# One step per slot: both products of the same 256 rows, with the table look-ups in front of the first

## The reference

```python
for e in range(E):                       # first mixture, E = 8
    mask = e_idx == e
    h = np.maximum(x[mask] @ w1[e], 0.0)         # [rows, 384] @ [384, 1024]
    out[mask] = gate_w[mask, None] * (h @ w2[e]) # [rows, 1024] @ [1024, 384]
...
for e in range(E):                       # second mixture
    for k in range(2):
        mask = top2[:, k] == e
        h = np.maximum(x[mask] @ w1[e], 0.0)
        out[mask] += top2_w[mask, k, None] * (h @ w2[e])
```

## Time and profile before

| | |
|---|---|
| median of 3 runs | 1062.32 us (1060.22 to 1062.54) |
| profiled execution, its own time | 1059.91 us |
| its span, first to last instruction | 1058.2 us |
| PE busy | 922.0 us (87%) |
| DVE, ACT, POOL busy | 529.5 us (50%), 226.3 us (21%), 355.8 us (34%) |
| mean granted TensorE clock | 0.955 of full speed |
| chain that ended last | PE 80%, DVE 10%, issue 6% |

### The profile page before, as it was taken

One profiled execution on the slowest core, in us unless ns is written; L12 is line 12 of the kernel. 1 busy time (PEld: TensorE's weight loads), 2 busy tenths in 40 slices (PEclk: granted clock), 3 DMA queues, 4 the chain that ended last, 5 costly groups with the idle time before them and its releaser, 6 DMA issues.

```text
span 1058.2 us, 22450 instructions
## 1 busy us (share of the span) xinstructions
PE 922.0 (87%) x7279; PEld 885.6 (84%) x7280; DVE 529.5 (50%) x946; ACT 226.3 (21%) x393; POOL 355.8 (34%) x358
## 2 busy tenths in 40 slices
PE   5999998999999987571699899998999999998893
PEld 5888887999999977561599899998989999998893
DVE  8889997863233342248543534335344353433431
ACT  2232251111011121143111313113122221311110
POOL 7333335043221321004443252433424334252321
PEclk9999998999999998875699999999999999999997
DMA  6666872083110111440343343423423434322221
GB/s 235 219 219 221 279 249 68 1 306 121 39 53 30 53 38 31 156 152 7 116 139 53 98 111 97 104 40 101 105 37 104 104 97 105 96 47 44 42 40 23
DMA packets 54089, 110.61 MB, mean 105 GB/s; under 512 B 8528, under 2 KB 35408, under 8 KB 54032
## 3 DMA queue, kind: packets, MB, share of 16 engines
q1 hardware_dynamic: 34656, 71.07, 20.2%
q0 software_dynamic: 15488, 33.92, 15.6%
q10 hardware_dynamic: 3888, 4.89, 1.3%
HBM read 84.05 MB, written 25.81 MB: 104 GB/s over the span
## 4 chain that ended last, share of the span: by engine, by line
PE 80%; DVE 10%; issue 6%; DMA 1%; POOL 1%; DVEq 0%; ACT 0%; POOLq 0%; ACTq 0%
PE ps L1655 22%; PE ps L1656 21%; PE ps L1657 21%; PE ps L1567 3%; PE ps L1527 2%; PE ps L1531 2%; PE ps L1473 2%; PE ps L1496 1%; DVE grow L890 1%; PE ps L1558 1%; PE ps L1581 1%; DVE scores L905 1%; PE ps L1592 1%; PE ps L1521 1%; DVE rest L875 1%
## 5 line engine op out<-in xcount | busy, mean ns | idle before, releaser
L1655 PE MATMUL ps<-x_hi,weights 128*128 128x256 f32 x984 | 278.9, 283 | 13.3 <-DVE weights L1086 10.9
L1657 PE MATMUL ps<-x_hi,weights 128*128 128x256 f32 x984 | 277.8, 282 | 0.0
L1656 PE MATMUL ps<-x_lo,weights 128*128 128x256 f32 x984 | 277.8, 282 | 0.0
L1655 PE MATMUL ps<-weights,hid_hi 128*128 (+1 forms) x616 | 216.5, 351 | 43.1 <-issue 38.6
L820 ACT ACTIVATE hid_hi<-ps 128x512 fp32r<-128x512 f32 x164 | 98.2, 599 | 575.8 <-PE ps L1657 572.7
L1656 PE MATMUL ps<-weights,hid_hi 128*128 (+1 forms) x616 | 209.0, 339 | 0.0
L1657 PE MATMUL ps<-weights,hid_lo 128*128 (+1 forms) x616 | 208.7, 339 | 0.0
L1364 DVE SCALAR_TENSOR_TENSOR hid_lo<-ps,hid_hi 128x512 fp32r<-128x512 f32 x164 | 112.7, 689 | 177.5 <-ACT hid_hi L820 170.0
L1655 PEld LDWEIGHTS ps<-x_hi,weights 128*128 128x128 f32 x984 | 187.4, 190 | 15.3 <-issue 15.2
L1657 PEld LDWEIGHTS ps<-x_hi,weights 128*128 128x128 f32 x984 | 187.3, 190 | 0.0
L1656 PEld LDWEIGHTS ps<-x_lo,weights 128*128 128x128 f32 x984 | 187.2, 190 | 0.0
(11 more groups left out here) (279 smaller groups left out, 1076.3 us busy)
## 6 DMA issues: line engine op xcount, KB each, us to landing
stage<-in_moe_w_dram SPq DMA_DIRECT2D x18, 1536.0 KB, 7.5
kv_in<-in_kv_T_dram SPq DMA_DIRECT2D x24, 512.0 KB, 5.5
kv_in<-in_kv_T_dram SPq DMA_DIRECT2D x24, 448.0 KB, 3.4
w_in<-in_w_T_dram SPq DMA_DIRECT2D x24, 258.5 KB, 4.1
out_dram<-zeros SPq DMA_DIRECT2D x25, 192.0 KB
x_rows<-y_tok ACTq DMA_DIRECT2D x24, 192.0 KB
stage<-moe_rows SPq DMA_DIRECT2D x6, 768.0 KB, 4.6
stage<-in_moe_w_dram SPq DMA_DIRECT2D x2, 768.0 KB
```

The costliest lines, as they stand in the source:

```text
L1655: pe.matmul(out_ps, hi, by_hi, start=first, stop=False)
L1656: pe.matmul(out_ps, hi, by_lo, start=False, stop=False)
L1657: return pe.matmul(out_ps, lo, by_hi, start=False, stop=final)
```

## The change

The step of TensorE becomes: look-ups of slot `s`, first product of slot `s`, then second product of the same slot. `run_of(s + 1)` is gone, since run and step now belong to the same slot; so there are two look-ups in a step where there were three. `hidden_high` and `hidden_low` of a slot move into that slot's step too, and the look-ups of ACT and DVE stand between two quarters. In a slot after which the run changes, both halves of w1's low part now come ahead of the second half of x. POOL has `split_next` ahead of the gather. The loops cover all sure slots, and the loop for the unsure ones is cut in two: the first part goes up to slot 13 (stage 1) or 27 (stage 2), the rest is entered only if more slots than that are used. The order of the small table operations in stage 1's first steps moves as well: `run_order` and `first_rows` come ahead of the second half of x, and `run_experts`, which releases SP's loads for the second run, comes after them. At the end of a stage there is now one more gather and one more turn and split, of a slot that is not used.

```diff
-        def slots(eng, l, step, peel=0):
-            pairs(eng, SURE[l] - 2, lambda j, u: step(j, u, lambda f: f()), peel)
+        def slots(eng, l, step, inner):
+            pairs(eng, SURE[l], step, PEEL[l], inner)
             eng.wait_ge(s_ends[l], 1)
             used = eng.value_load(used_i[l][0:1, 0:1], min_val=SURE[l], max_val=NS[l])
-            with eng.Fori(SURE[l] // 2 - 1, (NS[l] + 1) // 2) as j:
...
+            def maybe(j):
+                with eng.If(j * 2 < used):
+                    step(j, 0)
+                    with eng.If(j * 2 + 1 < used):
+                        step(j, 1)
+            soon = SURE[l] // 2 + l + 1
+            with eng.Fori(SURE[l] // 2, soon) as j:
+                maybe(j)
+            with eng.If(2 * soon < used):
+                with eng.Fori(soon, (NS[l] + 1) // 2) as j:
+                    maybe(j)
...
+                    if runs_from(l, s):                      # POOL
+                        split_next(s)
+                    rows_read(s + 2)
+                    gather(s + 3, s + 3, 1 - u)
                     scatter(s, j, u)
...
+                    hidden_high(s, 0)                        # ACT
+                    run = lookup(act, slot_run[l], s, E - 1)
+                    change, fresh = lookup(act, w1_now[l], s, 1), lookup(act, w2_now[l], s, 1)
+                    for q in range(1, 4):
+                        hidden_high(s, q)
+                    with act.If(change > 0):
...
+                    hidden_low(s, 0)                         # DVE
+                    hidden_low(s, 1)
...
+                        change, fresh = lookup(dve, w1_now[l], s, 1), lookup(dve, w2_now[l], s, 1)
+                    hidden_low(s, 2)
+                    split_x(s + 1, 1 - u, 0)
+                    hidden_low(s, 3)
+                    if runs_from(l, s):
+                        with dve.If(change > 0):
+                            for a in range(2):
+                                low_w1(l, run + 1, a)
+                        split_x(s + 1, 1 - u, 1)
+                        with dve.If(fresh > 0):
+                            low_w2(l, run + 1)
...
-                    run, two, run_next = run_of(s), second_of(s), run_of(s + 1)     # PE
+                    if not static:
+                        run, two = run_of(s), second_of(s)
+                    up(s, 0, run)
+                    up(s, 1, run)
...
+                    up(s, 2, run)
+                    up(s, 3, run)
+                    slot_turn(l, s + 1, j + u, 1 - u, 0)
...
                     down_second(s, 0, run, two)
                     down(s, 0, run, 0)
                     slot_turn(l, s + 1, j + u, 1 - u, 1)
                     down_second(s, 1, run, two)
                     down(s, 1, run, 0)
-                    for q in range(4):
-                        up(s + 1, q, run_next)
-                    slot_turn(l, s + 2, j + 1, u, 0)
-                pairs(pe, SURE[l] - 2, slot_step, PEEL[l], 1)
...
-                final = pe.value_load(last_i[l][0:1, 0:1], min_val=SURE[l] - 1, max_val=NS[l] - 1)
-                run, two = run_of(final), second_of(final)
-                for half in range(2):
-                    down_second(final, half, run, two)
-                    down(final, half, run, 0)
+                slots(pe, l, slot_step, 1)
```

157 lines of the change are left out of this document (53 added, 104 removed).

## The result

| | before | after |
|---|---|---|
| median | 1061.99 us (1060.22 to 1062.54, 4 runs) | 1005.81 us (1004.47 to 1007.93, 4 runs) |
| ratio to before | | 0.9476 (95%: 0.9455 to 0.9496) |
| span of the profiled execution | 1058.2 us | 1002.8 us |
| mean granted TensorE clock | 0.955 | 0.954 |

The kernel is 56.2 us faster by the medians, 55.4 by the spans; 45.1 had been forecast. The page of the changed kernel answers to the earlier trace rows with these lines: PE's share, the chain, and the first matmul of each product with its idle time.

The account below looks back on a forecast made before the run. TensorE was taken as the bound, standing still some 56 us. Terms 36.4 - 0.8 + 6.2 + 3.0 + 0 + 0.3 = 45.1 us off 1062.3 gave 1017 us; forecast 1014 to 1020 (0.55), whole range 1010 to 1029.

Parts of the forecast that it names:

- (a): TensorE's idle time ahead of the second products, 43.1 us, goes except 6.7 us at run changes: gain 36.4 us.
- (b): New TensorE idle time at the two entries to the loop of unsure slots, 0.4 us per stage: loss 0.8 us.
- (c): At the five run changes TensorE starts sooner behind the last Relu, 7.5 us (6.6 in stage 1): gain 6.2 us.
- (d): TensorE's clock stays higher at the stage ends: gain 2.0 us in stage 1 and 1.0 in stage 2.
- (e): Clock behind the waits for w1 at run changes: one drop in five as before, 0 us; bounds gain 1.6, loss 4.8.
- (f): POOL runs through fewer empty slots before it releases stage 2: gain 0.3 us, between 0 and 0.7.
- (g): No cost from ACT's and VectorE's look-ups between quarters, POOL's `split_next` ahead of the gather, or `run_experts` some 3 us later.
- 1 (stalls at the seam): Look-ups between second product and next first product only partly covered, edges and entries stall: 12 us, 1029 us; chance 0.17.
- 2 (clock drops): TensorE's clock drops in all four of stage 2's waits for w1: 4.8 us, 1022 us; chance 0.13.
- 3 (better covered): No gap at entries, no clock drop at run changes, stage 2 released earlier, more in (d): 3.8 us, 1013 us; chance 0.11.
- 4: VectorE's look-ups ahead of the third quarter's low part hold TensorE: 1103 us at 2 us per look-up; chance 0.02.

Follow-up runs that it names:

- old_orders: The changed kernel with POOL's `split_next` back behind the gather and, in changing slots, w1's second low half back behind x's second half: 1006.77 us, ratio 0.9478.

## Why the prediction was right and where it was wrong

The mechanism was right where most of the gain lies, in the look-ups and the run changes, and the size was off; the price of an entry and the reason given for the clock were wrong. Against the spans (55.4 us), term by term:

| term | forecast | measured |
|---|---|---|
| (a) stalls ahead of the second products | 36.4 | 43.7 |
| (b) new stalls at the two entries | -0.8 | 0 |
| (c) run changes | 6.2 | 7.3 |
| (d) clock at the stage ends | 3.0 | 3.7 |
| (e) clock at the run changes | 0 | -1.6 |
| (f) between the stages, and the end | 0.3 | 0.9 - 0.3 |
| rest | 0 | 1.7 |

**(a) is the step that failed.** "Gain 36.4" added up idle times as the rows print them. The idle time of a row counts from the modelled end of the instruction before. A turn is written as 0.49 us long, but without a stall the product behind it begins 0.25 us after its start, inside that length. A stall of 0.73 us is thus written as 0.50. The two starts were there to be subtracted in the earlier trace rows: 658.25 - 657.27 = 0.98 us for the stalled product, and 0.25 is what the changed kernel has in all its slots but one. Outside the changing slots the rows add up to 35.7 us, not 36.4 (the changing ones hold 7.4 us, not 6.7), and of the 33 stalls each is 0.24 us longer than its row: by the starts 43.7 us. The kernel with three look-ups put back shows it again (0.65 us, written as 0.40), and so does the kernel before with one moved (0.73 gained, 0.50 written). These 7.3 us are most of the 10.3 by which the spans miss the forecast.

**(b)** The lead at the seam was right, 3.1 us against the 2.98 read. Too dear was the entry: it was put at 1.55 us above a plain seam, and with five look-ups the two entries stall 0.9 and 1.4 us longer than a plain one (an edge 0.5, forecast 0.65). Taking off the three added look-ups of 0.64 us, the entries need some 2.6 and 3.1 us. The second is only just covered, so that it does not stall is partly luck. The "fixed number of matmuls" held: 3.1 us are 17 or 18 of 0.177 us at the seam, and at the old place it is as many. There the first look-up reads at 655.5, with three put back at 603.4, and the second product is due 2.0 us later, 0.25 us behind the turn's start: 15 matmuls of 0.119 us and the turn's three. The Trainium skill (TensorE: Matmul & The Clock Gate, "Architectural detail") gives 64 for the queue. 17 or 18 matmuls with as many weight loads are about 35, so its consequence, covered entries, came true, while its number is not what the trace shows.

**(c)** TensorE's start was right to 0.1 us at all five changes. The five changing slots went from 87.46 to 80.12 us together, 1.1 more than forecast. The forecast took the mean of 8.88 and 8.18 us for all four changes of stage 2, and the other two took 8.76 and 9.10 from the last Relu. The wait was forecast as 2.3 us and its row is 2.04 to 2.06 (2.2 by the starts), with 0.33 us (0.57 by the starts) ahead of the second half, where the branch waits for `hid_lo` as forecast. The cause is shown by moving the look-ups back: the chain from ACT's rounding through VectorE, free of both engines' look-ups. The order of w1 and x is worth next to nothing, as forecast.

**(d)** Last first product to result copy fell by 9.0 us in stage 1 and 4.1 in stage 2. 6.8 and 2.6 of that are the stalls, in (a); the clock gives 2.2 and 1.5. The forecast was 2.0 and 1.0.

**(e)** One more drop than before, 1.6 us. The rows show the granted clock over the first products behind the four waits for w1 in stage 2, in the changed kernel:

```profile
567.90:577.50 9.60, 9.60 (x70) 0.82 0.69 219
691.20:700.80 9.60, 9.60 (x70) 0.82 0.67 216
761.70:769.90 8.20, 8.20 (x71) 1.00 0.78 256
936.20:944.30 8.10, 8.10 (x71) 1.00 0.41 76
```

The forecast's reason, that waits of the length of 2.3 us had left the clock alone, was wrong: 2.04 and 2.05 us were followed by a drop, 2.06 and 2.05 were not, and before, 2.38 us were not the earlier trace rows. In the other kernels 1.76 us were, in that with three look-ups put back, and 2.78 us were not, in that with five at the seam. By length alone it can't be foretold in these kernels. Each drop cost 1.6 us.

**(f) and the rest.** From the result copy to stage 2 it is 0.9 us shorter in this profile, not 0.3; in the second profile of the changed kernel it is 88.5 us, no shorter than before, so no gain is shown here. Of the rest, 0.55 us are stage 2's first product, 10.14 instead of 10.69 us, and about 0.8 are 35 first products of 8.52 us that took 8.54 or 8.55 before. The cause of these is open, and so are the last few tenths.

**(g)** No cost was found in the places named: `old_orders` changes nothing, no second product waits for `hid_lo` but in the changing slots, and slot 3 of stage 1 does not wait for w2.

**The rivals.** 1 (stalls at the seam) did not come: no edge and no entry has any. 2 (clock drops) came in part, two of four in this profile, three in another. 3 (better covered) had the right sign at the entries and in (d), not in the clock drops, and its earlier stage 2 is not shown; its 3.8 us were too few because it took over the sum of (a). 4 did not come. The Trainium skill's rule on taken branches (Runtime: NRT & Kernel Launch, "Instruction fetch mechanics"), which had been put beside rival 1, does show in this case, at another place than thought: not at the loop edges, which the seam covers, but at the one far jump, 3.4 to 4.9 us. In the kernel with the cut loop the list of DMA queues (packets, MB, share) has one transfer of instructions from 412 to 416 us, while that jump lasted:

```profile
q8 instruction: 1, 0.02, 1.7%
```

The jump over a far shorter piece of program, 72 matmuls and their loads, stayed at 0.34 us or less.

## What to carry to other kernels

To size a stall on a pipelined engine, subtract starts and compare them with a place of the same kind that doesn't stall; the idle time in the row is too short by what the modelled end of the instruction before reaches into it. Put look-ups and branches where the queue holds the longest instructions, and find out how much is covered there from the sequencer's rows: from its first instruction at that place to the start that is due. Adding look-ups until it stalls tells the same, if the price of what was added is read from the rows too. Shortening a loop of empty passes by a jump over the rest saves nothing if work stands behind the jump; put the work ahead of it.

## What the runs showed of the hardware

VectorE's tiny `row_mix`, with both inputs in SBUF, takes 0.16 us, but when POOL's subtraction on w2 is already running, it does not end before that does. In the changed kernel, and then in the one with two buffers and x first:

```profile
582.98 0.96 DVE L1346 TENSOR_TENSOR row_mix<-sx,which 128x2 f32<-128x2 f32 x1 [2.36 <-PE ps L1545]
...
580.43 3.50 POOL L629 TENSOR_TENSOR weights<-stage,weights 128x1536 f32 x1 [2.53 <-ACT weights L772]
```

```profile
581.94 3.33 DVE L1352 TENSOR_TENSOR row_mix<-row_mix 128x1 f32 x1
...
581.75 3.51 POOL L629 TENSOR_TENSOR weights<-stage,weights 128x1536 f32 x1 [5.93 <-ACT weights L773]
```

582.98 + 0.96 is 583.94, and POOL ends at 583.93; 581.94 + 3.33 is 585.27, and POOL ends at 585.26. `x_hi` and `x_lo`, which read PSUM, kept their 0.56 us beside it (at 231.90 and 232.50 in the changed kernel). The Trainium skill (SBUF — State Buffer, "SBUF: two separate sides") says that a VectorE instruction with two SBUF inputs and a GpSimd one that reads SBUF exclude each other for the whole instruction; the trace agrees. With two buffers POOL's subtraction began at 591.18, 0.92 us before VectorE's low part of w1 ended, and took 4.28 instead of 3.50 us; so w1's low part and POOL's share of w2 in one slot hold each other up.

TensorE's sequencer was ahead of the array by 17 or 18 matmuls at both places, 3.1 us of the long ones and 2.0 us of the short ones. A look-up is mostly 0.75 us of the sequencer, 0.64 when the same one is repeated, and with the queue full it is free; a far jump was 3.4 to 4.9 us, and behind the last product of a stage it was free, since TensorE was not needed for longer than that. And behind waits of 2.04 to 2.06 us the clock of the next first product fell to the lower level or did not, from one wait to the next.
